# Evacuations split over two engines, squares of two frames on VectorE, no state products in block 0, idle matmuls at the start, a new order

## The chip, the cores and the metric

The kernel runs on one core of one Trainium2 chip. A core has TensorE (PE in the rows, its weight loads PEld), VectorE (DVE), ScalarE (ACT), GpSimd (POOL) and a queue engine (SP) that issues DMAs. The metric is the time of one execution on the device in microseconds (us); the median over executions counts.

## The reference: what is computed

Three stages in a row, all in fp32. First a gated linear attention over B=2, H=8, S=768, D=48, with a complex decay per position:

```python
mag = sqrt(a_re**2 + a_im**2); scale = minimum(mag, 0.999) / (mag + 1e-6)
for t in range(S):                       # state S_re, S_im: [B, H, D, D]
    S_re, S_im = ar*S_re - ai*S_im + k[t] v[t]^T, ar*S_im + ai*S_re
    y[t] = q[t] @ S_re
```

Then a mixture of experts over the 1536 tokens (y as rows of 384): a gate picks one of 8 experts, each relu(x w1) w2 with width 1024, up to a capacity. Last a network x w_in (2048 wide), a leaky relu with a slope per column, and w_out.

## The kernel before

**Attention as blocks.** The 768 positions are 6 blocks of 128, in 3 frames f of two blocks j. All logarithms and angles of the decay are summed over the positions of a frame by matmuls with triangular matrices: L_sums(f, j) and Th_sums(f, j) on TensorE, each two products of 384 columns. exps(f, j) turns the sums of logarithms into factors (ScalarE), scale(f, j) multiplies q and k with them (VectorE), phase(f, j) takes the angle to a fraction of a turn (VectorE), sin_cos(f, j) makes sine and cosine (ScalarE). Before that, the magnitude needs squares, logs, inverses, correction (ScalarE), tangent, clip_log, correct_log (VectorE) and angle (ScalarE), in four parts n: parts 0 and 1 are the two blocks of frame 0 (768 columns each), parts 2 and 3 are frames 1 and 2 (1536 columns each).

**Groups.** A block has 4 groups of four heads of one batch, so a frame has 8, numbered g. For a group: rotate(f, g) multiplies q and k with cosine and sine (VectorE, two instructions); transpose_group transposes both (TensorE, into banks TRQ and TRK); q_evacuate and k_evacuate copy these to SBUF; score_group multiplies them; mask_scores keeps the lower triangle (VectorE); apply_group multiplies the scores with v and adds q times the state from earlier blocks (the L1096 and L1099 products, 16 instructions each); add_group makes k^T v of the group for the state; state(f, u) adds it to w0 to give w1, or to w1 to give w2 (VectorE); shift_state takes w2 to the next frame. Two groups share one y, which y_evacuate(f, u) copies back. w0 of frame 0 is zero.

**Routing.** When a block's y is there, x_transpose(t), xT_evacuate(t) and tile_logits(t) make the gate's logits of 128 tokens, 12 in all, spread between the groups of frame 2. Then VectorE and TensorE route the tokens, GpSimd scatters the rows, and the experts and the network follow, bounded by TensorE. That part isn't touched.

**Order.** Each engine has its instructions in one list, written out by hand in the lines of calls: L496 to L590 for ScalarE, L778 to L885 for VectorE, L1136 to L1263 for TensorE. Engines wait for each other by counting semaphores; a wait holds everything behind it on that engine. ScalarE loads a table of functions when the kind changes (L422). ScalarE evacuates all but k of frame 0 and q of the first two groups, and squares both parts of frames 1 and 2 itself (L432, L433). One matmul call in fp32 is two instructions in the rows; a transpose is one. TensorE waits for the constants of GpSimd (`consts`) ahead of all. From frame 0 to frame 1 the last row of angles is carried: SP copies it by DMA after phase (carry_row), and carry_angle adds it on VectorE.

## Time and profile before

| | us |
|---|---|
| median of 3 runs (lowest, highest) | 519.65 (518.85, 520.82) |
| the profiled execution, its own time | 518.74 |
| its span in the profile | 516.7 |
| TensorE / VectorE / ScalarE busy over the span | 453.3 / 347.3 / 269.9 |
| attention and logits, to the first routing instruction | 146.1 |

The profile is of one execution. A view is one way of asking the trace: the table of stages gives busy time of each engine in stretches, the timeline gives instructions in order of time (start in us, duration in us, engine, line, output<-inputs, shapes, count, and in brackets how long the engine had been idle and what ended it), the groups give mean durations of equal instructions, and the chain goes back from the last instruction through what released each. A busy TensorE is pipelined: the pitch from start to start says more than the duration.

### The profile page before, as it was taken

Reading aid. Unit: us, or ns where it says so; the run is one execution under the profiler, and the core shown is the slowest. Engines: PE = TensorE matmul, PEld = TensorE weight load, DVE = VectorE, ACT = ScalarE, POOL = GpSimd, SP = SyncE. Lnnn points to the kernel's source line nnn. Section 1 sums busy time; section 2 is a strip of 40 time slices with the busy share of each in tenths; the row PEclk is TensorE's granted clock in tenths of the full one; section 3 lists DMA queues with packets and bytes.
Section 4 is the critical chain, followed back from the end, with each engine's and each line's share of the span. In section 5 each row is a group of like instructions: output and inputs, shape, how many; then the busy total and the mean of one; then the engine's idle time right before and its main releaser. Section 6 shows DMA issues by size and latency. Waiting matters only on the chain.

```text
span 516.7 us, 9892 instructions
## 1 busy us (share of the span) xinstructions
PE 453.3 (88%) x3712; PEld 409.2 (79%) x3712; DVE 347.3 (67%) x551; ACT 269.9 (52%) x425; POOL 40.1 (8%) x50
## 2 busy tenths in 40 slices
PE   0439989999940699999999989999999999999995
PEld 0227878899830499999999988999989999899985
DVE  2589898863350477777777767787747887478751
ACT  5999998564450466666666653333333333343312
POOL 3000000000037700000000000000030000200002
PEclk9969999999965699999999999999999999999999
DMA  8990000100015886667666672332333333210001
GB/s 310 421 369 2 4 3 3 3 3 3 3 31 200 277 266 196 178 204 217 204 198 198 182 225 67 110 105 91 93 122 115 99 99 108 94 68 1 0 1 63
DMA packets 27149, 63.75 MB, mean 123 GB/s; under 512 B 7894, under 2 KB 9430, under 8 KB 27100
## 3 DMA queue, kind: packets, MB, share of 16 engines
q1 hardware_dynamic: 25564, 58.34, 35.4%
q0 software_dynamic: 1536, 4.74, 2.4%
q8 instruction: 32, 0.52, 0.4%
q14 instruction: 17, 0.14, 0.1%
HBM read 58.28 MB, written 4.76 MB: 122 GB/s over the span
## 4 chain that ended last, share of the span: by engine, by line
PE 82%; DVE 5%; issue 4%; DMA 3%; POOL 3%; ACT 2%; SPq 0%; POOLq 0%; DVEq 0%; ACTq 0%
PE banks L1291 17%; PE banks L1289 17%; PE banks L1290 17%; PE banks L1299 8%; PE banks L1073 4%; PE banks L1300 4%; PE banks L1028 3%; PE banks L1096 2%; PE banks L1059 2%; POOL rows_by_slot L390 2%; PE banks L1099 2%; PE banks L1062 2%; DMA th<-a_im_rows 1%; PE banks L1109 1%; PE banks L1122 1%
## 5 line engine op out<-in xcount | busy, mean ns | idle before, releaser
L944 DVE TENSOR_TENSOR w_lo<-raw_early,w_hi 128x768 fp32r<-128x768 f32 x84 | 80.1, 957 | 30.0 <-ACT w_hi L599 29.0
L644 ACT ACTIVATE g_hi<-g_all 128x512 fp32r<-128x512 f32 x48 | 30.3, 632 | 119.0 <-DVE g_all L1001 119.0
L599 ACT ACTIVATE w_hi<-raw_early 128x768 fp32r<-128x768 f32 x84 | 70.3, 843 | 32.1 <-PE banks L1300 31.9
L1289 PE MATMUL banks<-w_hi,g_hi 128*128 128x384 f32 x192 | 65.1, 339 | 0.5 <-DVE g_lo L1003 0.5
L1291 PE MATMUL banks<-w_hi,g_lo 128*128 128x384 f32 x192 | 65.0, 339 | 0.0
L1290 PE MATMUL banks<-w_lo,g_hi 128*128 128x384 f32 x192 | 64.9, 338 | 0.0
L1299 PE MATMUL banks<-h_hi_lo,w_hi 128*128 128x448 f32 x192 | 64.0, 378 | 0.4 <-DVE h_hi_lo L964 0.4
L1003 DVE TENSOR_TENSOR g_lo<-g_all,g_hi 128x512 fp32r<-128x512 f32 x48 | 33.2, 693 | 44.2 <-ACT g_hi L644 44.2
L1289 PE MATMUL banks<-ys_hi,w_hi 128*128 128x512 f32 x144 | 56.1, 390 | 1.5 <-DVE ys_lo L978 1.5
L1291 PE MATMUL banks<-ys_hi,w_lo 128*128 128x512 f32 x144 | 57.1, 397 | 0.0
L1290 PE MATMUL banks<-ys_lo,w_hi 128*128 128x512 f32 x144 | 56.8, 394 | 0.0
L1289 PE MATMUL banks<-xs_hi,w_hi 128*128 x192 | 52.7, 275 | 0.1
L1290 PE MATMUL banks<-xs_lo,w_hi 128*128 x192 | 52.6, 274 | 0.0
L1291 PE MATMUL banks<-xs_hi,w_lo 128*128 x192 | 52.6, 274 | 0.0
L1300 PE MATMUL banks<-h_hi_lo,w_lo 128*128 128x224 f32 x192 | 50.8, 265 | 0.0
L999 DVE TENSOR_SCALAR g_neg<-banks,alpha 128x512 f32<-128x512 f32 x48 | 35.8, 747 | 7.7 <-PE banks L1291 7.6
L1299 PEld LDWEIGHTS banks<-h_hi_lo,w_hi 128*128 128x128 f32 x192 | 36.2, 189 | 3.9 <-DVE h_hi_lo L964 1.6
L1289 PEld LDWEIGHTS banks<-w_hi,g_hi 128*128 128x128 f32 x192 | 36.1, 188 | 3.4 <-DVE g_lo L1003 1.5
L1290 PEld LDWEIGHTS banks<-w_lo,g_hi 128*128 128x128 f32 x192 | 36.1, 188 | 2.0
L1289 PEld LDWEIGHTS banks<-xs_hi,w_hi 128*128 128x128 f32 x192 | 36.6, 191 | 1.0 <-issue 0.3
L399 POOL DMA_INDIRECT out_rows<-xq,tok_slot x12 | 11.8, 987 | 324.0 <-ACT xq L653 322.1
L1291 PEld LDWEIGHTS banks<-xs_hi,w_lo 128*128 128x128 f32 x192 | 36.9, 192 | 0.0
(146 smaller groups left out, 930.4 us busy)
## 6 DMA issues: line engine op xcount, KB each, us to landing
raw_early<-weights SPq DMA_DIRECT2D x84, 384.0 KB, 3.5
...
```

What stands on the lines that cost most here:

```text
L599: A(wh[:, slot, :], raw[slot], ACT.Copy).then_inc(w_hi, 1)
L644: A(gh[:, c % GBUF, :], gg[:, c % GBUF, :], ACT.Copy).then_inc(g_hi, 1)
L944: TT(wl[:, slot, :], raw[slot], wh[:, slot, :].bitcast(F32), ALU.subtract).then_inc(w_lo, 1)
L999: TS(gn[:, :], HM[c % HBUF][:, :], 0.0, alpha[:, i:i + 1], ALU.min, ALU.mult).then_inc(g_neg, 1)
L1003: TT(gl[:, c % GBUF, :], gg[:, c % GBUF, :], gh[:, c % GBUF, :].bitcast(F32), ALU.subtract).then_inc(g_lo, 1)
L1028: x = MM(to[:, b, :], lhsT=(through if j else beyond)[:, :], rhs=half(t, f, j, b), start=True, stop=True)
L1073: x = MM(SC[g % 2][:, c], lhsT=kT[:, g % 2, c], rhs=qT[:, g % 4, c], start=True, stop=True)
L1289: MM(o, lhsT=whi, rhs=mhi, start=first, stop=False)
L1290: MM(o, lhsT=whi, rhs=mlo, start=False, stop=False)
L1291: return MM(o, lhsT=wlo, rhs=mhi, start=False, stop=last)
L1299: MM(both, lhsT=whi, rhs=hs[:, slot, :, 0:n], start=first, stop=False)
L1300: return MM(o[:, 0:n], lhsT=wlo, rhs=hh[:, slot, 0:n], start=False, stop=last)
```

## The change

- Squares of parts 2 and 3 move from ScalarE to VectorE (re_im_squares). Those of parts 0 and 1 stay as they are.
- Evacuations: of 24 q, 24 k, 12 y and 12 xT, VectorE makes 8, 9, 8 and 4 (before 2, 8, 0, 0) and ScalarE the rest.
- apply_group of the first block (f = 0, j = 0, four groups) leaves out the products with the state, which is zero.
- 23 calls of idle_matmuls on TensorE: 16 ahead of all sums, one after Th_sums(0, 0), six after L_sums(0, 0). Each is four products of the identity with itself into a bank that is overwritten later. Th_sums(0, 0) now comes before L_sums(0, 0), and L_sums(0, 1) after the first transposes.
- ScalarE does part 0 to the end before part 1, with one table load more in all.
- Waits are added in rotate, shift_state, state and add_group.
- The order of all three lists is new, mainly in frames 0 and 1; add_group comes earlier in TensorE's list. The diff shows the lists up to frame 1; in the rest, too, single calls change places.

```diff
--- before.py
+++ after.py
@@ -426,12 +426,6 @@
                 act.wait_ge(a_dma[n], 32)
                 A(part(lr, n), part(th, n), ACT.Square).then_inc(im_squared, 1)
 
-            def squares(n):
-
-                act.wait_ge(a_dma[n], 32)
-                A(part(lr, n), part(th, n), ACT.Square)
-                A(part(t1, n), part(aa, n), ACT.Square).then_inc(squared_later, 1)
-
             def logs(n):
                 table(LOGS)
                 act.wait_ge(u_ready, n + 1)
@@ -495,96 +489,75 @@
 
             table(LOGS)
             square(0)
+            logs(0)
+            inverses(0)
             square(1)
-            logs(0)
+            correction(0)
+            angle(0)
             logs(1)
-            inverses(0)
             inverses(1)
-            correction(0)
+            exps(0, 0)
             correction(1)
-            angle(0)
             angle(1)
-            squares(2)
-            exps(0, 0)
+            sin_cos(0, 0)
+            logs(2)
+            q_evacuate(0, 0)
             exps(0, 1)
-            sin_cos(0, 0)
+            inverses(2)
+            k_evacuate(0, 2)
+            correction(2)
             sin_cos(0, 1)
-            logs(2)
-            inverses(2)
-            q_evacuate(0, 2)
-            correction(2)
-            squares(3)
-            q_evacuate(0, 3)
             angle(2)
+            k_evacuate(0, 3)
+            exps(1, 0)
+            k_evacuate(0, 4)
+            y_evacuate(0, 0)
             q_evacuate(0, 4)
-            exps(1, 0)
-            q_evacuate(0, 5)
-            y_evacuate(0, 0)
             exps(1, 1)
             logs(3)
             q_evacuate(0, 6)
             sin_cos(1, 0)
             q_evacuate(0, 7)
-            y_evacuate(0, 1)
             inverses(3)
             k_evacuate(1, 0)
-            q_evacuate(1, 0)
             correction(3)
-            y_evacuate(0, 2)
+            k_evacuate(1, 1)
             q_evacuate(1, 1)
-            k_evacuate(1, 1)
+            y_evacuate(0, 3)
             sin_cos(1, 1)
             k_evacuate(1, 2)
-            y_evacuate(0, 3)
             q_evacuate(1, 2)
             angle(3)
...
@@ -677,9 +650,14 @@
                 dve.wait_ge(re_squared, n + 1)
                 TT(part(t1, n), part(t1, n), part(lr, n), ALU.add).then_inc(u_ready, 1)
 
+            def re_im_squares(n):
+                dve.wait_ge(a_dma[n], 32)
+                TT(part(lr, n), part(th, n), part(th, n), ALU.mult)
+                TT(part(t1, n), part(aa, n), part(aa, n), ALU.mult).then_inc(squared_by_dve, 1)
+
             def squared_sum(n):
 
-                dve.wait_ge(squared_later, n - 1)
+                dve.wait_ge(squared_by_dve, n - 1)
                 TT(part(t1, n), part(t1, n), part(lr, n), ALU.add).then_inc(u_ready, 1)
 
             def scale(f, j):
@@ -735,6 +713,8 @@
                     dve.wait_ge(trig_ready, 2 * f + (j + 1))
                     dve.wait_ge(scaled, 2 * f + (j + 1))
                 dve.wait_ge(added, ROT_FREE + 8 * f + (g + 1 - 4))
+                if 8 * f + g >= 4:
+                    dve.wait_ge(transposed, 8 * f + (g + 1 - 4))
                 at = j * BW + b * UW + h * D
                 trig = cs[:, :, at:at + G4 * D].rearrange("p c (h d) -> p c h d", d=D)
                 for dst, src in ((qt, rows(f, j, b)), (kt, half(kk, f, j, b))):
...
@@ -742,16 +722,25 @@
                            heads(src)[:, None, h:h + G4, :].to_broadcast([P, 2, G4, D]), trig, ALU.mult)
                 x.then_inc(rot_ready, 1)
 
+            def q_evacuate(f, g):
+                dve.wait_ge(transposed, 8 * f + (g + 1))
+                if 8 * f + g >= 4:
+                    dve.wait_ge(applied, QT_FREE + 8 * f + (g + 1 - 4))
+                dve.tensor_copy(qT[:, g % 4, :], TRQ[0:DP, :]).then_inc(q_out, 1)
+
             def k_evacuate(f, g):
-                if f >= 1:
-                    return
                 dve.wait_ge(transposed, 8 * f + (g + 1))
                 dve.wait_ge(scored, KT_FREE + 8 * f + (g + 1 - 2))
                 dve.tensor_copy(kT[:, g % 2, :], TRK[0:DP, :]).then_inc(k_out, 1)
 
-            def first_q_evacuate(g):
-                dve.wait_ge(transposed, g + 1)
-                dve.tensor_copy(qT[:, g, :], TRQ[0:DP, :]).then_inc(q_out, 1)
+            def y_evacuate(f, u):
+                dve.wait_ge(applied, QT_FREE + 8 * f + (2 * u + 2))
+                dve.tensor_copy(rows(f, u // 2, u % 2), YB[:, 0:UW]).then_inc(y_out, 1)
+
+            def xT_evacuate(t):
+                dve.wait_ge(xT_made, t + 1)
+                dve.wait_ge(logits_made, XT_FREE + t + 1 - 2)
+                dve.tensor_copy(xT[:, t % 2, :], XB[:, 0:DM]).then_inc(xT_out, 1)
 
             def mask_scores(f, g):
                 dve.wait_ge(scored, KT_FREE + 8 * f + (g + 1))
@@ -764,6 +753,8 @@
                 c = slice((u % 2) * UW, (u % 2 + 1) * UW)
                 src, dst = (w0, w1) if u < 2 else (w1, w2)
                 dve.wait_ge(added, ROT_FREE + 8 * f + (2 * u + 2))
+                if f >= 1 and u < 2:
+                    dve.wait_ge(applied, QT_FREE + 8 * (f - 1) + (2 * u + 6))
                 TT(dst[:, c], UB[0:DP, 0:UW], src[:, c], ALU.add).then_inc(state_out, 1)
 
             def shift_state(f, b):
@@ -772,116 +763,138 @@
                 if b == 0:
                     dve.wait_ge(hop_ready, f + 1)
                 dve.wait_ge(state_out, U_FREE + 6 * f + (5 if b else 3))
+                dve.wait_ge(applied, QT_FREE + 8 * f + (2 * b + 2))
                 TT(heads(w0[:, c]), heads(w2[:, c]), hop[:, 1, h][:, :, None].to_broadcast([DP, H, D]),
                    ALU.mult).then_inc(state_out, 1)
 
             re_square(0)
             abs_square(0)
             re_square(1)
+            tangent(0)
+            clip_log(0)
             abs_square(1)
-            tangent(0)
+            correct_log(0)
+            re_im_squares(2)
+            phase(0, 0)
+            squared_sum(2)
             tangent(1)
-            clip_log(0)
             clip_log(1)
-            correct_log(0)
+            scale(0, 0)
+            re_im_squares(3)
+            rotate(0, 0)
+            phase(0, 1)
             correct_log(1)
-            squared_sum(2)
-            phase(0, 0)
-            scale(0, 0)
-            phase(0, 1)
-            scale(0, 1)
-            rotate(0, 0)
             rotate(0, 1)
             k_evacuate(0, 0)
-            first_q_evacuate(0)
             rotate(0, 2)
+            state(0, 0)
+            rotate(0, 3)
             k_evacuate(0, 1)
-            first_q_evacuate(1)
+            q_evacuate(0, 1)
+            scale(0, 1)
             mask_scores(0, 0)
-            k_evacuate(0, 2)
-            rotate(0, 3)
+            clip_log(2)
             mask_scores(0, 1)
+            q_evacuate(0, 2)
             tangent(2)
+            correct_log(2)
+            state(0, 1)
+            q_evacuate(0, 3)
             rotate(0, 4)
-            clip_log(2)
-            k_evacuate(0, 3)
-            correct_log(2)
-            state(0, 0)
-            mask_scores(0, 2)
-            k_evacuate(0, 4)
             rotate(0, 5)
             rotate(0, 6)
+            mask_scores(0, 2)
+            rotate(0, 7)
+            carry_angle(1, 0)
             squared_sum(3)
-            state(0, 1)
             mask_scores(0, 3)
-            carry_angle(1, 0)
+            q_evacuate(0, 5)
+            scale(1, 0)
             k_evacuate(0, 5)
-            scale(1, 0)
+            state(0, 2)
             phase(1, 0)
-            rotate(0, 7)
             k_evacuate(0, 6)
-            carry_angle(1, 1)
+            y_evacuate(0, 1)
             mask_scores(0, 4)
             mask_scores(0, 5)
-            state(0, 2)
+            k_evacuate(0, 7)
+            carry_angle(1, 1)
             rotate(1, 0)
             rotate(1, 1)
-            k_evacuate(0, 7)
-            phase(1, 1)
+            mask_scores(0, 6)
+            mask_scores(0, 7)
+            y_evacuate(0, 2)
+            q_evacuate(1, 0)
             hop_factors(1)
             rotate(1, 2)
             shift_state(0, 0)
-            mask_scores(0, 6)
...
@@ -1031,6 +1044,11 @@
             def first_frame(f):
                 return isinstance(f, int) and f == 0
 
+            def idle_matmuls():
+
+                for _ in range(4):
+                    MM(YB[:, 0:P], lhsT=ident[:, :], rhs=ident[:, :], start=True, stop=True)
+
             def L_sums(f, j):
                 pe.wait_ge(lnr_ready, parts(f, j))
                 if not first_frame(f):
@@ -1090,18 +1108,20 @@
                     pe.wait_ge(y_out, Y_FREE + 4 * f + g // 2)
                     pe.wait_ge(state_out, U_FREE + 6 * f + (b + 1 if j else -2 * (1 - b)))
                 w = w1 if j else w0
+                first = f == 0 and j == 0
                 for i in range(G4):
                     h = g % 2 * G4 + i
                     for r in ROW_HALVES:
-                        MM(YB[r, h * D:(h + 1) * D], lhsT=sc[:, g % 2, i * P + r.start:i * P + r.stop],
-                           rhs=values(f, g, i), start=True, stop=False)
-                    for r in ROW_HALVES:
+                        x = MM(YB[r, h * D:(h + 1) * D], lhsT=sc[:, g % 2, i * P + r.start:i * P + r.stop],
+                               rhs=values(f, g, i), start=True, stop=first)
+                    for r in ROW_HALVES if not first else ():
                         x = MM(YB[r, h * D:(h + 1) * D], lhsT=qT[:, g % 4, i * P + r.start:i * P + r.stop],
                                rhs=w[:, b * UW + h * D:b * UW + (h + 1) * D], start=False, stop=True)
                 x.then_inc(applied, 1)
 
             def add_group(f, g):
                 values_here(f, g)
+                pe.wait_ge(rot_ready, 8 * f + (g + 1))
                 if g % 2 == 0:
                     pe.wait_ge(state_out, U_FREE + 6 * f + (-1, 1, 2, 3)[g // 2])
                 for i in range(G4):
@@ -1133,62 +1153,85 @@
                                start=(k == 0), stop=(k == KB - 1))
                 x.then_inc(logits_made, 1)
 
+            idle_matmuls()
+            idle_matmuls()
+            idle_matmuls()
+            idle_matmuls()
+            idle_matmuls()
+            idle_matmuls()
+            idle_matmuls()
+            idle_matmuls()
+            idle_matmuls()
+            idle_matmuls()
+            idle_matmuls()
+            idle_matmuls()
+            idle_matmuls()
+            idle_matmuls()
+            idle_matmuls()
+            idle_matmuls()
+            Th_sums(0, 0)
+            idle_matmuls()
             L_sums(0, 0)
-            L_sums(0, 1)
-            Th_sums(0, 0)
+            idle_matmuls()
+            idle_matmuls()
+            idle_matmuls()
+            idle_matmuls()
+            idle_matmuls()
+            idle_matmuls()
             Th_sums(0, 1)
             transpose_group(0, 0)
+            add_group(0, 0)
+            L_sums(0, 1)
+            add_group(0, 1)
             transpose_group(0, 1)
+            add_group(0, 2)
             score_group(0, 0)
             transpose_group(0, 2)
             score_group(0, 1)
+            add_group(0, 3)
             apply_group(0, 0)
-            add_group(0, 0)
+            apply_group(0, 1)
+            score_group(0, 2)
             transpose_group(0, 3)
-            score_group(0, 2)
-            add_group(0, 1)
-            apply_group(0, 1)
+            L_sums(1, 0)
+            add_group(0, 4)
             transpose_group(0, 4)
-            L_sums(1, 0)
-            add_group(0, 2)
-            add_group(0, 3)
             score_group(0, 3)
-            transpose_group(0, 5)
+            add_group(0, 5)
             L_sums(1, 1)
             apply_group(0, 2)
+            transpose_group(0, 5)
             score_group(0, 4)
+            apply_group(0, 3)
             Th_sums(1, 0)
             transpose_group(0, 6)
-            add_group(0, 4)
-            add_group(0, 5)
-            apply_group(0, 3)
+            add_group(0, 6)
             score_group(0, 5)
+            add_group(0, 7)
             transpose_group(0, 7)
+            apply_group(0, 4)
+            apply_group(0, 5)
             score_group(0, 6)
+            score_group(0, 7)
+            transpose_group(1, 0)
             Th_sums(1, 1)
-            add_group(0, 6)
-            apply_group(0, 4)
-            transpose_group(1, 0)
-            apply_group(0, 5)
-            score_group(0, 7)
-            add_group(0, 7)
+            apply_group(0, 6)
             transpose_group(1, 1)
+            apply_group(0, 7)
             score_group(1, 0)
-            apply_group(0, 6)
+            add_group(1, 0)
             transpose_group(1, 2)
-            add_group(1, 0)
-            apply_group(0, 7)
+            add_group(1, 1)
             score_group(1, 1)
             L_sums(2, 0)
-            add_group(1, 1)
             apply_group(1, 0)
+            score_group(1, 2)
             apply_group(1, 1)
+            add_group(1, 2)
+            add_group(1, 3)
             transpose_group(1, 3)
-            add_group(1, 2)
-            score_group(1, 2)
-            add_group(1, 3)
+            apply_group(1, 2)
             L_sums(2, 1)
...
```

## Rows read from the trace of the kernel before

**Rows 1.** Table of stages: PE, PEld, DVE, ACT, POOL busy us, PEclk, DMA, GB/s.

```profile
70.00:80.00 10.00, 10.00 (x175) 9.20 (x176) 9.93 (x16) 9.16 (x13) 0.00 (x0) 1.00 0.02 4
...
130.00:140.00 10.00, 10.00 (x175) 9.03 (x176) 3.03 (x6) 4.22 (x9) 0.00 (x0) 1.00 0.01 2
```

**Rows 2.** Timeline of VectorE at the end of the logits.

```profile
146.11 0.26 DVE L896 COPY logit<-banks 128x96 f32<-128x96 f32 x1 [4.49 <-PE banks L1132]
```

**Rows 3.** Timeline at 65 to 67 us, VectorE and TensorE.

```profile
65.20 1.27 DVE L759 TENSOR_TENSOR scores<-banks,upto 128x512 f32<-128x512 f32 x2
...
66.02 1.13 PE L1073 MATMUL banks<-qT,kT 112*128 112x128 f32 x8 [1.61 <-DVE scores L759]
```

**Rows 4.** Timeline of TensorE, 92 to 98 us.

```profile
92.44 1.56 PE L1028 MATMUL banks<-th,upto_per_turn 128*128 128x384 f32 x4
...
94.80 0.32 PE L1096 MATMUL banks<-vv,scores 128*64 128x48 f32 x4
...
95.77 0.22 PE L1109 MATMUL banks<-vv,k_rot 128*64 128x48 f32 x1
...
96.33 2.05 PE L1073 MATMUL banks<-qT,kT 112*128 112x128 f32 x16
98.31 0.26 PE L1109 MATMUL banks<-vv,k_rot 128*64 128x48 f32 x1
```

**Rows 5.** Timeline of TensorE's weight loads, 19 to 42 us.

```profile
19.42 0.50 PEld L1028 LDWEIGHTS banks<-lr,after 128*128 128x128 f32 x2 [19.42 <-issue]
...
22.79 0.33 PEld L1028 LDWEIGHTS banks<-lr,upto 128*128 128x128 f32 x1 [0.31 <-issue]
23.43 0.33 PEld L1028 LDWEIGHTS banks<-lr,upto 128*128 128x128 f32 x1 [0.31 <-issue]
23.89 1.16 PEld L1028 LDWEIGHTS banks<-th,after_per_turn 128*128 128x128 f32 x4
25.18 1.16 PEld L1028 LDWEIGHTS banks<-th,upto_per_turn 128*128 128x128 f32 x4
33.97 0.69 PEld L1059 LDWEIGHTS banks<-ident,q_rot 128*112 128x112 f32 x4 [7.63 <-DVE k_rot L741]
...
38.90 1.83 PEld L1073 LDWEIGHTS banks<-qT,kT 112*128 112x128 f32 x8
40.77 0.41 PEld L1059 LDWEIGHTS banks<-ident,q_rot 128*112 128x112 f32 x4
```

**Rows 6.** Timeline of ScalarE at its start.

```profile
4.30 1.28 ACT L422 ACT_TABLE_LOAD   x1 [4.30 <-POOL prior L376]
```

**Rows 7.** Timeline of VectorE, 25 to 28 us.

```profile
25.70 0.96 DVE L711 TENSOR_SCALAR cos_sin<-banks 128x768 f32<-128x768 f32 x1 [0.30 <-PE banks L1028]
...
27.57 0.95 DVE L689 TENSOR_TENSOR xq<-xq,aa 128x768 f32<-128x768 f32 x1
```

**Rows 8.** Groups, 0 to 150 us: busy us, mean ns, idle before.

```profile
L741 DVE TENSOR_TENSOR k_rot<-kk,cos_sin 128x384 f32<-128x384 f32 x24 | 13.2, 550 | 0.0
...
L750 DVE COPY kT<-banks 112x512 f32<-112x512 f32 x8 | 5.5, 683 | 2.5 <-PE banks L1062 2.5
...
L695 DVE TENSOR_TENSOR th<-th,aa 128x1536 f32<-128x1536 f32 x2 | 3.5, 1749 | 0.0
...
L700 DVE TENSOR_SCALAR lr<-lr 128x1536 f32<-128x1536 f32 x2 | 1.9, 950 | 0.0
...
L479 ACT ACTIVATE qT<-banks 112x512 f32<-112x512 f32 x22 | 13.0, 589 | 6.9 <-PE banks L1062 6.8
```

**Rows 9.** Chain of waits: start us, us, what.

```profile
14.31 0.73 ACT aa L445
...
61.66 2.57 DMA xT<-th
```

**Rows 10.** Timeline of VectorE, 84 to 100 us, two rows with idle.

```profile
86.84 0.69 DVE L759 TENSOR_TENSOR scores<-banks,upto 128x512 f32<-128x512 f32 x1 [2.27 <-PE banks L1073]
...
94.11 0.96 DVE L711 TENSOR_SCALAR cos_sin<-banks 128x768 f32<-128x768 f32 x1 [1.05 <-PE banks L1028]
```

155 lines of the change are left out of this document (77 added, 78 removed).

## Prediction

> **What bounds the kernel now.** I read the table of stages first, since busy shares are means over stages. From 70 to 140 us TensorE is busy all the time; VectorE and ScalarE are nearly full beside it at 70 to 80 and down to a third or so at 130 to 140 [rows 1]. So the attention stage has two halves. The second is bounded by TensorE: the last logits land at 146.11 and nothing else is due before them [rows 2]. The seam is at 66.02: the timeline has TensorE idle for 1.61 us until VectorE's masked scores, and I found no idle of it after that up to the logits [rows 3]. Before the seam it is VectorE's order that sets the pace.
>
> From this follows the way to count: the end of the stage is the moment at which TensorE stops waiting, plus the work that is then left on it. What follows the logits (routing, experts, network) isn't touched, so a shift of that end is the shift of the kernel.
>
> TensorE's own prices at full clock, from start to start in the timeline [rows 4]: a running sum of four instructions and a transposed group 2.36 us together (92.44 to 94.80), an applied group of 32 instructions 0.97 (94.80 to 95.77), an added group 0.56 (95.77 to 96.33), and two score groups 1.98 (96.33 to 98.31), so 0.99 for one, which is four matmuls in eight instructions.
>
> **The idle matmuls: their price.** A call of idle_matmuls is four 128x128 products in fp32, the same shape and count as a score group but for 128 rows instead of 112. So it costs 0.99 us at full clock [rows 4] and 1.87 us at half clock (38.90 to 40.77) [rows 5]. They can start when the constants are there, at 4.30 [rows 6]. The weight loads of the first sums start 0.64 us apart (22.79 to 23.43) and after 23.89 four of them take 1.29 (to 25.18), 0.32 each: the engine ran at 1.2 GHz from its first work at 19.42 to about 23.8, and at 2.4 GHz thereafter [rows 5]. That is 4.4 us. The sixteen calls in front therefore take 4.4 us for the first 2.35 and 13.65 x 0.99 = 13.5 us for the rest, and end at 22.2. This is late: the angles that Th_sums(0, 0) needs are ready at about 15.6, by ScalarE's new order (square and logs to 9.1, table 10.4, inverses 11.9, square 12.7, correction 13.4, table 14.7, arctangent 15.6; a table load 1.28 [rows 6], 768 columns 0.74 behind one another and 0.83 behind a wait, as the chain shows them [rows 9]). TensorE takes its instructions in order, so Th_sums(0, 0) runs from 22.2 to 23.6. Bounds: if the clock is full from the start, 16 x 0.99 ends at 20.1, 2.1 earlier; if it takes as long to rise as in the second cold stretch, whose half-speed work begins at 33.97 and ends at 40.77 (6.8 us) [rows 5], it ends at 23.3, 1.1 later. I take 22.2, since that stretch has gaps and the first one has none.
> The page "TensorE: Matmul & The Clock Gate" of the Trainium skill (section "What's actually happening") says that the throttled state is the default and activity releases it. By that rule the idle calls pay: the sums, two transposed groups and a score group that ran at half speed in this trace would run at full speed, some 5 us of TensorE's time. The sum here gives them nothing, since VectorE is last in that stretch.
>
> **VectorE from there on.** One of its instructions costs its duration less about 0.08, because the next starts before it ends: two masks of 0.69 take 1.27 [rows 3]. A phase takes 1.87 (25.70 to 27.57), a scale two pieces of 0.95, so 1.73 [rows 7]; a rotation 2 x 0.47 = 0.93; an evacuation 0.61 for 512 columns, and 0.47 for 384, as a state; 1536 columns 1.67, 768 columns 0.87; a clip of 1536 columns 0.87, of 768 half of it [rows 7, 8].
> From 23.6: phase(0, 0) 1.9, squared_sum(2) 1.7, tangent(1) 0.9, clip_log(1) 0.5, scale(0, 0) 1.7, re_im_squares(3) 2 x 1.67 = 3.35. Sum 10.1: rotate(0, 0) starts at 33.7, beside 32.9 before. The two squares of frame 1, re_im_squares(2), lie at 15.3 to 18.7 while VectorE would wait for the angles anyway: nothing, as long as the idle run lasts that long.
> From 33.7 to the end of mask_scores(0, 4): 8 rotations 7.4, phases (0, 1) and (1, 0) 3.8, scales (0, 1) and (1, 0) 3.5, eight evacuations of 512 columns 4.9, three states 1.4, one y 0.5, five masks 3.0, tangent(2), correct_log(2) and squared_sum(3) 5.0, clip_log(2) and correct_log(1) 1.7, carry_angle(1, 0) 0.9. Sum 32.1: it ends at 65.8, and the trace of before has the same mask end at 65.8, too (65.20 and 0.60) [rows 3]. What is taken off VectorE there (three k evacuations) comes back as q and y evacuations and as squares.
> Does ScalarE keep up? With an added table load of 1.28 [rows 6] and without the squares the cosines of (0, 0) come at 32.8 (needed 33.7), the exponentials of (0, 1) at 40.7 (42.5), the cosines of (0, 1) at 49.5 (51.5). Slack 1 to 2 us: none is last. The carried row takes 2.57 us from phase(1, 0) [rows 9]; that ends at 64.2, so it lands at 66.8, and carry_angle(1, 1) is due at 67.0. Covered, by little.
>
> **TensorE from there on.** At 66.0 it starts apply_group(0, 4). At 66.0 in the kernel before it starts score_group(0, 6). What is then left differs by two added groups: before, add_group(0, 6) and (0, 7) are still to come, after they are done. That is 2 x 0.56 to 0.6 = 1.2 us less. I walked the rest of the order with the prices above, and TensorE has no wait: its inputs are there 0.6 to 1.5 us ahead (least at L_sums(2, 0) and Th_sums(2, 1), 0.6 us). After about 105 VectorE has time to spare again.
> **State products of block 0.** 4 groups x 16 instructions, half of 0.97 each: 1.9 us less on TensorE. All four lie before 66 us, where it waits for VectorE: nothing.
> **Evacuations moved.** 6 q, 1 k, 8 y and 4 xT go to VectorE (7 x 0.61 + 12 x 0.47 = 9.9 us), the squares add 4 x 1.67 = 6.7; ScalarE is relieved by about as much. An evacuation of 112x512 takes 683 ns on VectorE and 589 on ScalarE [rows 8]. Beyond frame 0 they lie in VectorE's gaps, which are two of 2.27 and 1.05 us between 84 and 94 [rows 10] and large ones after 105.
> The Trainium skill speaks against that part: "ScalarE is closer to PSUM, VectorE is closer to SBUF" (page "ScalarE: Activation LUTs", section "Step-by-step: what each stage is for"). The trace agrees, by 0.09 us for one evacuation. By the rule the nineteen moved copies are a loss of 1.8 us, where the sum has none because TensorE covers them.
> **New waits.** rotate waits for the transposes of four groups before, shift_state and state for applied groups, add_group for its own rotation. Each is met 1 us or more earlier by the orders above: nothing.
>
> **Sum.** 0 for VectorE's chain, -1.2 for the two groups already done. The profiled execution took 518.74 us (span 516.7), so 517.5; the median of the runs shown is 0.9 higher, 519.65, so 518.4.
>
> **Rivals.**
> *The idle run ends sooner.* If the clock is full from the start, everything from Th_sums(0, 0) on is 2.1 us earlier, because VectorE's order carries it one to one: -3.3, 516.4. For it: no row shows the pace before 19.42. Against: the first work there is ran at half pace [rows 5]. If an idle product were one instruction, like a transpose, the run would end before 15.6 and ScalarE's inverses would be last: rotate(0, 0) at 28.9, 4.8 earlier, -6.0 in all, 513.7. Against: every fp32 product written with matmul stands as two in the counts.
> *VectorE is late in frame 1 (slower than before).* From 66 to 98 its order has no gap left, where before it idled 3.3 us at two waits for TensorE [rows 10]. Now five evacuations there (y and q) each wait for a product that has just ended. If the old waits stay (3.3) and the five add 0.4 each (2.0), 5.3 us less the slack of 0.6 reach TensorE: 4.7 later, 523.1. It decides from 1.8 us of VectorE waits on, where the gain is gone.
> *The clock falls again* between 34 and 50, where TensorE has work for about three quarters of the time. L_sums(0, 1) and the groups before it then take 3.1 us more, ScalarE's slack takes 2: with what follows +1.5, 519.9.
> *It doesn't do what it says:* the state products and the clock give nothing because they aren't on the path. That is the forecast itself.
>
> **How the numbers follow.** Forecast 0.50, idle run at full clock 0.20, the one-instruction case 0.05, VectorE late 0.15, clock falls 0.10. Within 0.5% (2.6 us, about what a measurement of this kernel can tell from no change) lie the forecast but for its lower edge, the fallen clock and a mild form of the late VectorE: 0.58. Faster by more: the two cases of the shorter run and that edge, 0.28. Slower by more: 0.14. The range goes from 515.0 (the full clock, and 1.4 us that I overcharged VectorE's 42 us) to 522.0 (the long rise of the clock, +1.1, and half of the late VectorE, +2.4).
>
> **What would show it.** The start of Th_sums(0, 0) at 22.2: much earlier means the price or the clock of the idle calls was wrong. rotate(0, 0) at 33.7 without idle before it on VectorE from 23.6. The mask of (0, 4) ending at 65.8. TensorE's timeline without idle from 66 on: idle before a score or transposed group of frame 1, released by VectorE, is the slower rival. Half clock between 34 and 50 is the third. If the logits land later than 146.1 with all of these right, the pitches of TensorE have changed.

## The result and the profile after

The kernel after takes 516.34 us in the median of 8 runs (515.51 to 517.72), against 519.64 (518.21 to 520.82) of 8 runs of the kernel before. The ratio is 0.9938 with an interval of [0.9923, 0.9953]: 3.3 us, or 0.6%, faster. The prediction was 518.4 with a range of 515.0 to 522.0: the time lies in the range, but the gain of 3.3 us is over two and a half times the 1.2 forecast.

The profiled execution took 516.6 us, its span is 514.6, so 2.1 less than before. The page gives busy time of each engine over the span:

```profile
span 514.6 us, 10165 instructions
PE 471.6 (92%) x3832; PEld 428.6 (83%) x3832; DVE 363.7 (71%) x574; ACT 257.8 (50%) x403; POOL 40.2 (8%) x50
```

The table of stages (busy us of PE, PEld, DVE, ACT, POOL with the number of instructions, granted clock, DMA share, GB/s):

```profile
34.00:38.00 4.00, 3.00 (x24) 1.92 (x23) 3.97 (x8) 3.38 (x4) 0.00 (x0) 0.77 0.89 343
38.00:42.00 4.00, 4.00 (x47) 2.77 (x46) 2.58 (x7) 2.89 (x6) 0.00 (x0) 0.80 0.03 9
...
70.00:80.00 10.00, 10.00 (x142) 8.37 (x141) 9.93 (x16) 9.45 (x13) 0.00 (x0) 1.00 0.01 2
130.00:140.00 10.00, 10.00 (x194) 9.23 (x193) 5.21 (x9) 1.69 (x3) 0.00 (x0) 1.00 0.01 3
```

TensorE is full in both late stretches, as before [rows 1]; at 130 to 140 work has gone from ScalarE to VectorE (5.21 and 1.69, before 3.03 and 4.22). The first pair shows the granted clock between 34 and 42 us. It is below full there, though higher than in the kernel before:

```profile
34.00:38.00 4.00, 2.53 (x11) 2.14 (x12) 2.89 (x6) 3.97 (x4) 0.00 (x0) 0.50 0.93 360
38.00:42.00 4.00, 4.00 (x26) 3.97 (x25) 2.27 (x5) 3.97 (x4) 0.00 (x0) 0.65 0.01 3
```

Timeline of VectorE and TensorE (start us, us, engine, line, what, idle before and what ended it) at the seam and at the last logits:

```profile
65.15 1.28 DVE L748 TENSOR_TENSOR scores<-banks,upto 128x512 f32<-128x512 f32 x2
65.89 0.32 PE L1115 MATMUL banks<-vv,scores 128*64 128x48 f32 x4
...
143.76 0.26 DVE L909 COPY logit<-banks 128x96 f32<-128x96 f32 x1 [4.52 <-PE banks L1152]
```

The seam is where it was (65.15, before 65.20 [rows 3]), and TensorE has no idle before its row at 65.89. The logits come at 143.76, before at 146.11 [rows 2]: 2.35 us earlier. Nearly all of it was gained behind the seam, where 77.87 us are left (65.89 to 143.76), before 80.09 (66.02 to 146.11).

One thing is different at the seam itself. Before, TensorE stood idle there for 1.61 us. Now the last wait that its timeline shows ahead of the seam is this one:

```profile
52.43 0.26 PE L1129 MATMUL banks<-vv,k_rot 128*64 128x48 f32 x1 [0.44 <-DVE k_rot L721]
```

From 52.4 us on TensorE is full, and VectorE is full beside it. I keep the word seam for the mask at 65.15, so that kernels can be compared, but TensorE bounds the stage from somewhat earlier on (e3_state_back below shows it).

**The beginning.** TensorE's timeline:

```profile
4.34 16.71 PE L1050 MATMUL banks<-ident 128*128 128x128 f32 x128 [4.34 <-POOL prior L376]
20.89 1.46 PE L1041 MATMUL banks<-th,after_per_turn 128*128 128x384 f32 x4
22.18 1.05 PE L1050 MATMUL banks<-ident 128*128 128x128 f32 x8
23.07 1.46 PE L1041 MATMUL banks<-lr,after 128*128 128x384 f32 x4
...
33.40 0.65 PE L1077 MATMUL banks<-ident,q_rot 128*112 128x128 f32 x4 [2.22 <-DVE k_rot L721]
...
36.12 2.89 PE L1041 MATMUL banks<-lr,upto 128*128 128x384 f32 x4 [0.18 <-DVE lr L683]
```

A call of idle_matmuls is 0.89 us where it stands alone (22.18 to 23.07), not 0.99, so the angle sums run from 20.9 and not from 22.2. Then TensorE idles, the mean granted clock from 34 to 38 us is 0.77 (table above), and L_sums(0, 1) at 36.12 takes 2.89 us, where four instructions of the same shape took 1.46 at 20.89.

VectorE's timeline, with the two ends of that:

```profile
22.38 0.96 DVE L689 TENSOR_SCALAR cos_sin<-banks 128x768 f32<-128x768 f32 x1 [3.91 <-PE banks L1041]
...
32.33 0.55 DVE L721 TENSOR_TENSOR q_rot<-xq,cos_sin 128x384 f32<-128x384 f32 x1
...
39.96 0.56 DVE L758 TENSOR_TENSOR w<-banks,w 112x384 f32<-112x384 f32 x1 [1.42 <-PE banks L1131]
```

rotate(0, 0) starts at 32.33 (forecast 33.7). state(0, 0) at 39.96 has waited 1.42 us for add_group(0, 1), which stands behind L_sums(0, 1) on TensorE. So 1.3 us gained are 1.4 lost, and the seam doesn't move.

**Behind the seam.** The chain of waits, before (L1073 score groups, L1028 sums) and after (L1091, L1041), in pieces of start us, us, what:

```profile
72.05 1.09 PE banks L1073 x8
74.75 0.89 PE banks L1073 x8
80.35 1.29 PE banks L1028 x4
87.40 1.49 PE banks L1028 x4
```

```profile
75.26 1.09 PE banks L1091 x8
79.64 1.29 PE banks L1041 x4
87.17 1.49 PE banks L1041 x4
88.66 0.89 PE banks L1091 x8
```

A score group has two prices in both kernels. It is 0.89 behind products whose weights fill 112 or 128 columns (scores, transposes, sums) and 1.09 behind those whose weights are 64 or 48 columns (apply, add, logits: "128*64" in the timeline); a sum is 1.29 or 1.49. A change back from narrow to full weights costs 0.20 us. By the lists of calls TensorE makes 32 such changes behind the seam before and 28 after.

### The profile page after: what moved, and what is told of

Same layout as the page of the kernel before. It is cut to its first block, busy times and chain, and to the rows that moved or that the text cites. A ratio compares the mean times of both kernels' runs of the same rounds, so it can differ in the third digit from the quotient of the medians.

```text
span 514.6 us, 10165 instructions
## 1 busy us (share of the span) xinstructions
PE 471.6 (92%) x3832; PEld 428.6 (83%) x3832; DVE 363.7 (71%) x574; ACT 257.8 (50%) x403; POOL 40.2 (8%) x50
## 4 chain that ended last, share of the span: by engine, by line
PE 79%; DVE 5%; issue 3%; POOL 3%; DMA 1%; ACT 1%; DVEq 0%; POOLq 0%; SPq 0%; ACTq 0%
PE banks L1332 16%; PE banks L1334 16%; PE banks L1333 16%; PE banks L1342 8%; PE banks L1091 4%; PE banks L1343 4%; PE banks L1041 2%; PE banks L1115 2%; POOL rows_by_slot L390 2%; PE banks L1077 2%; PE banks L1118 2%; PE banks L1080 2%; PE banks L1129 1%; PE banks L1326 1%; PE banks L1142 1%
```

## The experiments

Each kernel was timed in three rounds beside the kernel before. Three moments of its profile are in this table: rotate(0, 0), the mask that is the seam, and the last logits. The last columns are the median and the ratio to the kernel before as it was timed beside each.

| kernel | rotate(0, 0) | seam | logits | seam to logits | us | ratio |
|---|---|---|---|---|---|---|
| before | 32.90 | 65.20 | 146.11 | 80.91 | 519.64 | |
| after | 32.33 | 65.15 | 143.76 | 78.61 | 516.34 | 0.9938 [0.9923, 0.9953] |
| e1_no_idle | 31.48 | 63.42 | 142.02 | 78.60 | 515.20 | 0.9914 [0.9887, 0.9942] |
| e2_ten_ahead | 32.23 | 63.85 | 142.46 | 78.61 | 515.65 | 0.9928 [0.9904, 0.9953] |
| e4_keep_clock | 32.52 | 63.84 | 142.45 | 78.61 | 515.57 | 0.9912 [0.9884, 0.9940] |
| e5_ten_and_clock | 32.19 | 65.98 | 145.22 | 79.24 | 516.88 | 0.9931 [0.9909, 0.9954] |
| e3_state_back | 32.88 | 65.92 | 144.85 | 78.93 | 516.35 | 0.9946 [0.9929, 0.9962] |
| e8_fewer_switches | 32.31 | 64.95 | 141.69 | 76.74 | 513.63 | 0.9895 [0.9878, 0.9911] |
| e9_evac_back | 32.28 | 64.95 | 143.71 | 78.76 | 517.03 | 0.9958 [0.9943, 0.9972] |
| e11_sp_first | 28.31 | 59.63 | 138.24 | 78.61 | 510.83 | 0.9844 [0.9828, 0.9861] |
| e6_before_adds | 33.01 | 65.79 | 145.50 | 79.71 | 518.13 | 0.9982 [0.9966, 0.9999] |
| e7_before_idle | 32.84 | 64.15 | 145.06 | 80.91 | 518.92 | 0.9993 [0.9977, 1.0010] |
| e10_squares_act | 31.89 | 63.22 | 141.83 | 78.61 | 514.84 | 0.9926 [0.9900, 0.9953] |
| e12_all | 28.31 | 59.64 | 136.38 | 76.74 | 509.74 | 0.9827 [0.9798, 0.9856] |

Read the column from seam to logits first. It is 78.61 within 0.01 us in six kernels whose seams lie between 59.6 and 65.2 us. So the way to count of the prediction holds: the time is where TensorE stops waiting, plus the work left on it. Three kernels with the same order of TensorE behind the seam stand a little off: e9_evac_back (78.76), e3_state_back (78.93) and e5_ten_and_clock (79.24), where VectorE waits 0.90 us for the carried row at 98.64.

The moments are sharper than the medians. Behind the seam they repeat to 0.01 us in those six; ahead of it they don't: four kernels with the same order up to rotate(0, 0) have it between 32.28 and 32.52, and a fifth (e3_state_back) at 32.88. Of the kernels made from the kernel after, only e8_fewer_switches, e11_sp_first and e12_all have ratios whose intervals lie apart from its own. For the others a difference to it rests on the moments of one profile each. The rest of the span, from the logits on, which no kernel changes, varied from 369.8 to 371.6 us over these fourteen profiles, and one profile's time can't be told from another's within that.

**Without the idle matmuls.** All 23 calls are taken out.

```diff
-            idle_matmuls()      (23 times)
```

> The changed kernel without any of the 23 calls of idle_matmuls. In the trace of the changed kernel the 16 calls in front end at 20.89 us, while the angles that Th_sums(0, 0) needs are ready at about 15.6, and VectorE works without a gap from phase(0, 0) at 22.38 to 38.5. Theory 1 (the idle run delays the start of VectorE's chain, and the clock is worth little in that stretch): Th_sums(0, 0) starts at 15.6 at half clock, rotate(0, 0) at about 28.5 instead of 32.3, 3.8 us earlier; the transposes and sums of block 0 at half clock take about 1.5 us of it back; 2.3 us faster than the changed kernel, 514.0 us. Rival (the idle calls pay, because they keep the clock at 2.4 GHz until the real work comes): without them sums, transposes and scores of block 0 run at half clock and VectorE waits for them; slower than the changed kernel by 1 to 5 us, 517.5 to 521.

Measured: 515.20 us, and the logits at 142.02, 1.7 earlier than with the calls. TensorE and VectorE:

```profile
15.69 2.90 PE L1041 MATMUL banks<-th,after_per_turn 128*128 128x384 f32 x4 [15.69 <-ACT th L449]
...
26.40 0.96 DVE L667 TENSOR_TENSOR xq<-xq,aa 128x768 f32<-128x768 f32 x1 [2.81 <-SPq L299]
```

The angles are there at 15.69, as the prediction had it (15.6). At half clock the sums take twice as long, and yet they come earlier: the calls in front had held them for 5.2 us (15.69 to 20.89). Little of that arrives. The second row is a surprise: scale(0, 0) waits 2.81 us for SP, so rotate(0, 0) is only 0.85 us earlier than in the kernel after, and not 3.8. The other 0.9 comes from the wait at state(0, 0), which is 0.52 us instead of 1.42, because L_sums(0, 1) takes 2.11 us instead of 2.89. The measured time lies between the theory (514.0) and the rival (517.5 or more). By the medians the calls cost 1.1 us, but the two intervals overlap; by the logits it is 1.7.

**Ten calls in front instead of sixteen.**

```diff
-            idle_matmuls()      (6 of the 16 ahead of Th_sums(0, 0))
```

> The changed kernel with 10 calls of idle_matmuls ahead of the sums instead of 16. In the changed kernel 20 instructions run at half clock to 8.6 us and the rest 0.113 us apart, so 10 calls should end at about 15.6, just when the angles are ready. Theory 1: Th_sums(0, 0) at 15.7 instead of 20.9; VectorE's phase(0, 0) at 18.4 (behind its squares of part 2) instead of 22.4; rotate(0, 0) at about 28.5 instead of 32.3; the logits end 3.6 us earlier; 512.7 us. Rival: ScalarE becomes last (its inverses end at 21.35 in any case, and its exponentials, angle and cosines follow from there) and holds the rest of the chain: 1 us or less faster than the changed kernel, 515.5.

Measured: 515.65, and rotate(0, 0) at 32.23, not at 28.5. The sums did start early (15.78) and at full clock (1.46 us). VectorE then stops:

```profile
27.14 0.96 DVE L667 TENSOR_TENSOR xq<-xq,aa 128x768 f32<-128x768 f32 x1 [3.82 <-SPq L299]
```

What SP does meanwhile, in its timeline of the kernel after:

```profile
17.90 9.18 SPq L295 DMA_DIRECT2D raw_early<-weights  x6
```

SP announces that q, k and v of frame 0 have landed (`qkv_here`, L299), and only after it has issued six loads of expert weights, which hold it until 27.1. In the kernel after scale(0, 0) starts at 27.25, right behind, so this bound stood exactly where VectorE's own order came to it and was visible in no idle time. Neither theory had it; the rival's 515.5 is met for another reason than its own.

The logits are 1.3 us earlier all the same. With rotate(0, 0) where it was, this comes from the clock: TensorE's transposes ran at half clock (granted 0.50 from 30 to 34 us), but the clock was up again during L_sums(0, 1), and from 38 to 42 us it was 1.00 (0.80 in the kernel after).

```profile
36.21 1.80 PE L1041 MATMUL banks<-lr,upto 128*128 128x384 f32 x4
38.66 0.56 DVE L758 TENSOR_TENSOR w<-banks,w 112x384 f32<-112x384 f32 x1 [0.21 <-PE banks L1131]
```

L_sums(0, 1) took 2.89 us in the kernel after, and VectorE's wait at state(0, 0) was 1.42; here they are 1.80 and 0.21.

**The clock kept up.** Two idle calls after Th_sums(0, 1) and one after transpose_group(0, 0), into the first bank of scores.

```diff
             Th_sums(0, 1)
+            idle_in_scores()
+            idle_in_scores()
             transpose_group(0, 0)
+            idle_in_scores()
             add_group(0, 0)
```

> The changed kernel with three more calls of idle matmuls, into a scores bank that is still free: two between Th_sums(0, 1) and transpose_group(0, 0), where TensorE waits 2.2 us for the rotation, and one after transpose_group(0, 0). In the changed kernel the granted clock is 0.77 at 34 to 38 us and 0.80 at 38 to 42, L_sums(0, 1) takes 2.89 us instead of 1.46, ScalarE waits for it until 39.11 and VectorE stands idle 1.42 us before state(0, 0). Theory (the fallen clock costs these 1.4 us): with the clock kept up L_sums(0, 1) takes 1.4 us, VectorE's idle time goes, all that follows is 1.2 to 1.4 us earlier; 515.0 us. Rival (VectorE waits there for other reasons, or the time is given back later where TensorE alone is bound): no change, 516.3.

Measured: 515.57 us, logits at 142.45, 1.3 earlier than after. TensorE and its clock:

```profile
36.32 1.56 PE L1041 MATMUL banks<-lr,upto 128*128 128x384 f32 x4
```

```profile
34.00:38.00 4.00, 3.85 (x42) 2.80 (x41) 3.97 (x7) 3.60 (x5) 0.00 (x0) 1.00 0.93 353
```

The sums of logarithms take 1.56 and not 2.89, and the 1.42 us of VectorE's wait at state(0, 0) are gone. That was the fallen clock, as the theory had it. (The ratio, 0.9912 with an interval up to 0.9940, doesn't separate this kernel from the kernel after.)

**Both.**

```diff
-            idle_matmuls()      (6 of the 16)
+            idle_in_scores()    (3, as above)
```

> Both edits together: 10 idle calls in front and three more around transpose_group(0, 0). Theory: the two add up, since one moves the start of VectorE's chain and the other takes a hole out of it: 3.6 + 1.3 = 4.9 us faster than the changed kernel, 511.4 us. Rival (ScalarE is last from then on, since its slack was 1 to 2 us): no faster than the better of the two alone, 512.7.

Measured: 516.88, logits at 145.22. Both expectations missed by 4 us or more. TensorE:

```profile
33.26 1.10 PE L1082 MATMUL banks<-ident,q_rot 128*112 128x128 f32 x4 [4.07 <-DVE k_rot L721]
34.16 1.06 PE L1085 MATMUL banks<-ident,k_rot 128*112 128x128 f32 x4
35.01 1.91 PE L1055 MATMUL banks<-ident 128*128 128x128 f32 x8
37.87 2.27 PE L1041 MATMUL banks<-lr,upto 128*128 128x384 f32 x4
```

TensorE ran dry early, waited 4.07 us for VectorE, which waited for SP, and lost its clock. The idle call meant to keep it then took 1.91 us in front of the sums, and state(0, 0) waited 2.38 us. Only the three calls tell this kernel from e2_ten_ahead, whose seam lies at 63.85: they made it 2.13 us later. An idle call behind a long wait, with the clock already down, was a cost and no help. By the ratio (0.9931) the kernel is as fast as the kernel after.

**The state products of block 0 back.**

```diff
-                first = f == 0 and j == 0
+                first = False
```

> The changed kernel with the state products of block 0 back (32 matmul calls on zeros, 64 instructions). Theory, as in the prediction: they lie before 66 us, where TensorE waits for VectorE, so they cost next to nothing. Looked at closely, the groups (0, 2) and (0, 3) lie at 57 to 60.2 us, where TensorE's order is without idle up to Th_sums(1, 0); 1.0 us later there makes phase(1, 0) some 0.4 us later: 0.0 to 0.5 slower than the changed kernel, 516.3 to 516.8. Rival: all of it is on the path, half of four applied groups of 1.07, 1.9 to 2.1 us slower, 518.3.

Measured: 516.35, the ratio 0.9946 against 0.9938 for the kernel after: the same within the intervals. In its profile the logits are 1.1 later. A part of that is not the products': SP's announcement was late in that execution, and VectorE waited for it.

```profile
27.80 0.96 DVE L667 TENSOR_TENSOR xq<-xq,aa 128x768 f32<-128x768 f32 x1 [0.66 <-SPq L299]
```

TensorE's starts, here and in the kernel after, separate the two. At the first product of apply_group(0, 2) this kernel is 0.26 us late (57.28 and 57.02). Then come the products of the groups (0, 2) and (0, 3):

```profile
61.32 1.56 PE L1041 MATMUL banks<-th,upto_per_turn 128*128 128x384 f32 x4
66.98 0.32 PE L1115 MATMUL banks<-vv,scores 128*64 128x48 f32 x4
```

In the kernel after these two rows stand at 60.13 and 65.89. So it is 1.19 late behind the two groups, 1.09 late at the seam and 1.09 late at the logits: of some 0.93 us of products 0.83 came through. Those of the first two groups (45 to 47 us) did not: ahead of them and at apply_group(0, 2) the delay is the same 0.25. The rival, that the 1.9 us of products come back in full, is out. But they aren't free either: 0.8 us by the profile, more than the 0 to 0.5 expected. The ratio is too coarse to show it.

**Eighteen evacuations of frames 1 and 2 back to ScalarE.**

```diff
-            q_evacuate(1, 0)    (on VectorE; with it 3 more q, 4 k, 6 y, 4 xT)
+            q_evacuate(1, 0)    (the same 18 calls on ScalarE)
```

> The changed kernel with the eighteen evacuations of frames 1 and 2 that VectorE makes (4 q, 4 k, 6 y, 4 xT) back on ScalarE; frame 0 and TensorE's order stay. Theory: from 66 us on TensorE is never late, so who evacuates doesn't matter: 516.3, within 0.4. Rival 1 (VectorE is too full from 66 to 100 and delays TensorE by pieces that the timeline doesn't show): 1 us faster. Rival 2 (split evacuation is what keeps TensorE fed, since ScalarE alone hands q and k over later): 1 to 2 us slower, with idle of TensorE before transposed and score groups.

Measured: 517.03, and the logits at 143.71, as after (143.76). VectorE gets idle time back (1.53 us at 92, for one), and TensorE's timeline shows none. From seam to logits it is 0.15 more. The median is 0.7 us above that of the kernel after, within the intervals. So the split is worth 0.15 us by the profile, and nothing that the ratios can tell.

**Fewer changes of weight width.** Frame 2 of TensorE's list in another order, with 8 changes from narrow to full weights from x_transpose(1) on instead of 16; a few evacuations change places with it.

```diff
             tile_logits(0)
-            x_transpose(2)
             add_group(2, 1)
+            x_transpose(2)
             score_group(2, 0)
...
             apply_group(2, 2)
+            apply_group(2, 3)
+            tile_logits(7)
+            x_transpose(8)
             transpose_group(2, 6)
-            apply_group(2, 3)
-            x_transpose(8)
-            transpose_group(2, 7)
-            tile_logits(7)
             x_transpose(9)
...
```

> The changed kernel with another order of TensorE's list in frame 2 only: added groups, applied groups and logits follow one another where they can, so that there are 8 changes from products of 64 columns of weights (apply, add, logits) to full ones (scores, transposes, sums) from x_transpose(1) on, where there were 16. The y of (2, 1) and the xT of 8 are evacuated one place earlier; the work is the same. Both traces show a score group at 1.09 us behind a group of the first kind and at 0.89 behind one of the second, a sum at 1.49 and 1.29, a transposed group at 1.02 and 0.88. Theory: a change costs about 0.17 us, so this is 8 x 0.17 = 1.4 us faster than the changed kernel, 514.9; the logits at 142.4 instead of 143.8. Rival (the difference lies in how ends are modelled, or the new order makes TensorE wait for evacuations): no faster, 516.3 or more.

Measured: 513.63, ratio 0.9895. From seam to logits 76.74 us instead of 78.61: 1.87 for eight changes, 0.23 each, with the same products.

```profile
141.69 0.26 DVE L909 COPY logit<-banks 128x96 f32<-128x96 f32 x1 [3.89 <-PE banks L1152]
```

That is somewhat more than expected, and none of it lies ahead of the seam. TensorE shows no wait in that stretch in either kernel, so it is not a wait that went.

**SP announces first.** With ten calls in front and the clock kept:

```diff
+            sp.wait_ge(qkv_dma[0], 48)
+            sp.sem_inc(qkv_here, 1)
             for i in range(AHEAD):
                 sp.dma_start(raw[i], w_in[i, :, :]).then_inc(w_dma[i], 16)
...
-            for f in range(NF):
+            for f in range(1, NF):
```

> The kernel with 10 idle calls ahead and three more around transpose_group(0, 0), and with one move on SP: it waits for q, k and v of frame 0 and announces them before it issues the six loads of weights, not after. With 10 calls VectorE stood idle 3.8 us before scale(0, 0), until SP's count at 27.1, right after SP had issued the last of these loads (16.99 and 10.06 us later). Theory: the data had long landed and only SP's order held the count back; then scale(0, 0) starts at about 23.4, rotate(0, 0) at 28.5, all that follows comes 3.8 us earlier and the clock stays up through L_sums(0, 1): logits at 142.45 - 3.8 = 138.7, 511.8 us. Rival (the transfers themselves land at 26 to 27, all sixteen DMA engines being full until 37): as with the late count, 515.6 to 516.9.

Measured: 510.83, logits at 138.24 (expected 138.7). Against e5_ten_and_clock this differs by SP's order alone, and is 7.0 us earlier at the logits and 0.0087 lower in the ratio (4.5 us):

```profile
23.24 0.95 DVE L669 TENSOR_TENSOR xq<-xq,aa 128x768 f32<-128x768 f32 x1
...
28.31 0.55 DVE L723 TENSOR_TENSOR q_rot<-xq,cos_sin 128x384 f32<-128x384 f32 x1
```

```profile
29.39 0.65 PE L1084 MATMUL banks<-ident,q_rot 128*112 128x128 f32 x4 [0.19 <-DVE k_rot L723]
...
32.11 1.56 PE L1043 MATMUL banks<-lr,upto 128*128 128x384 f32 x4
```

VectorE has 0.30 us of idle time (at 78.69) from there to 87 us, TensorE waits 0.19 us where it had waited 4.07, and its clock stays.

**The added groups alone, in the kernel before.** add_group(0, 6) and (0, 7) go ahead of score_group(0, 6), with state(0, 2) earlier on VectorE so that they can.

```diff
+            state(0, 2)
             carry_angle(1, 1)
             mask_scores(0, 4)
             mask_scores(0, 5)
-            state(0, 2)
...
             transpose_group(0, 7)
+            add_group(0, 6)
+            add_group(0, 7)
             score_group(0, 6)
             Th_sums(1, 1)
-            add_group(0, 6)
...
-            add_group(0, 7)
```

> The kernel before with one step of the change alone: state(0, 2) goes ahead of carry_angle(1, 1) on VectorE, and add_group(0, 6) and (0, 7) go ahead of score_group(0, 6) on TensorE, into the 1.6 us in which it waits for the masked scores until 66.02. Theory, as in the prediction: work that is moved into that hole no longer stands behind it; 2 x 0.56 = 1.1 us faster than before. Rival (the hole is needed for the transfer of the carried row and moves with it, or VectorE's state comes later than the hole): no change.

Measured: 518.13, ratio 0.9982 [0.9966, 0.9999], 0.9 us. From seam to logits 79.71 instead of 80.91, so 1.20. The seam itself is 0.6 later. VectorE waits for the carried row as long as before (1.11 us, before 1.16); it is the row that comes later:

```profile
64.92 0.95 DVE L721 SCALAR_TENSOR_TENSOR th<-xT,th 1x768 f32<-1x768 f32 x1 [1.11 <-DMA xT<-th]
65.79 1.27 DVE L759 TENSOR_TENSOR scores<-banks,upto 128x512 f32<-128x512 f32 x2
```

phase(1, 0) starts 0.17 later than before (59.85 and 59.68), and the DMA of the row took 3.0 us from its issue to landing instead of 2.6. The edit touches neither.

**The idle matmuls alone, in the kernel before.** Fourteen calls ahead of L_sums(0, 0).

```diff
+            idle_matmuls()      (14 times)
             L_sums(0, 0)
             L_sums(0, 1)
```

> The kernel before with 14 calls of idle_matmuls ahead of L_sums(0, 0) and nothing else; they should end at about 19.0 us, just ahead of the sums at 19.45. Theory: the sums then run at full clock and end some 2 us earlier, but ScalarE comes to the exponentials only at 24.9, behind its squares and a table load, and VectorE to the phase behind squared_sum at 25.4: 0 to 0.3 us faster than before. Rival (idle matmuls pay by themselves): the 2 us of the sums go through to the end, 517.2 to 517.7.

Measured: 518.92, ratio 0.9993 [0.9977, 1.0010]. The time says nothing measurable. Its profile has the seam 1.05 earlier:

```profile
63.27 0.95 DVE L721 SCALAR_TENSOR_TENSOR th<-xT,th 1x768 f32<-1x768 f32 x1 [0.25 <-DMA xT<-th]
```

Before, the same instruction waited 1.16 us for the carried row. The first two sums took 2.90 and 2.23 us before and 1.46 and 1.45 here, but phase(1, 0) is only 0.14 us earlier (59.54 and 59.68). The rest of the 1.05 is the row's DMA, from issue to landing, before and here:

```profile
xT<-th SPq DMA_DIRECT2D x1, 3.0 KB, 2.6
xT<-th SPq DMA_DIRECT2D x1, 3.0 KB, 1.7
```

So the idle calls gave at most 0.14 us, inside the 0 to 0.3 expected, and 0.9 is the transfer of one small row, whose time differs from profile to profile.

**The squares of part 3 on ScalarE,** in the idle time it has after inverses(1).

```diff
             inverses(1)
+            squares(3)
...
-            re_im_squares(3)
```

> The changed kernel with the squares of part 3 (frame 2) on ScalarE, in its idle time of 3.3 us before the exponentials of (0, 0); VectorE makes those of part 2 only. Theory: VectorE has 3.35 us less ahead of rotate(0, 0), which then waits for the cosines at 31.45 instead of standing at 32.33: 0.9 us faster, 515.4, logits at 142.9. Rival 1 (ScalarE is pushed and hands over the exponentials later): no gain. Rival 2 (VectorE's whole 3.35 us come through): 513.0.

Measured: 514.84, logits at 141.83, 1.9 earlier than after. VectorE and ScalarE:

```profile
31.89 0.56 DVE L728 TENSOR_TENSOR q_rot<-xq,cos_sin 128x384 f32<-128x384 f32 x1 [2.78 <-ACT cos_sin L474]
```

```profile
22.30 1.48 ACT L432 ACTIVATE lr<-th 128x1536 f32<-128x1536 f32 x1 [0.98 <-DMA th<-a_im_rows]
```

VectorE sheds 3.35 us of squares and gets 0.44 of it: ScalarE's squares begin at 22.30, when the rows of a have landed, and with their 2.9 us ahead of them the cosines become last. The other 1.4 come from TensorE: it waited 1.73 us instead of 2.22 before the first transposes, kept the clock (1.00 from 34 to 38), and state(0, 0) didn't wait.

**All of it:** e11_sp_first with the order of e8_fewer_switches.

> The kernel with SP's announcement first, 10 idle calls ahead and the clock kept, and the order of frame 2 with fewer changes between kinds of products. Theory: the two gains lie in different stretches (before 60 us and after 100 us) and add up: logits at 138.2 - 2.0 = 136.2, 508.8 us. Rival (with TensorE 4 us earlier, VectorE and ScalarE are late in frame 2 for the tighter order): 509.5 to 510.8, with idle of TensorE after 100 us.

Measured: 509.74, ratio 0.9827 [0.9798, 0.9856], the fastest of all.

```profile
136.38 0.26 DVE L911 COPY logit<-banks 128x96 f32<-128x96 f32 x1 [3.89 <-PE banks L1159]
```

Its seam is that of e11_sp_first, its work behind it that of e8_fewer_switches (76.74): in the moments the two gains add up. The median lies 0.9 above the 508.8 expected, in the rival's range, but TensorE shows none of the rival's idle time after 100 us. The interval overlaps that of e11_sp_first.

## Why the prediction was right and wrong

**Right: the bound and the way to count.** The stage ends when TensorE stops waiting plus what is left. The column from seam to logits shows it. The moment itself moved, though: in the new order TensorE's last wait is at 52.4, not at 66. TensorE had no wait for VectorE in frame 1: the slower rival was wrong. The 1.8 us of waits from which it decides never came: VectorE's one wait of over 0.3 us between 66 and 98 is 0.58.

**Right: VectorE's chain.** 32.1 us were forecast from rotate(0, 0) to the end of mask_scores(0, 4). The trace has 32.33 to 65.75, so 33.4, of which 1.42 is the wait at state(0, 0): 32.0. The 10.1 us ahead of it were 9.95 (22.38 to 32.33).

**Right in the main: the added groups.** Forecast 1.2, and 1.20 in e6_before_adds between seam and logits. It has one change of width fewer as well, 31 for 32, so the groups alone are 1.0.

**Right: the evacuations, priced at nothing.** e9_evac_back has the logits 0.05 us apart. The Trainium skill says (page "ScalarE: Activation LUTs", section "Step-by-step: what each stage is for") that ScalarE is closer to PSUM. The copies here agree (512 columns took 589 ns on ScalarE and 683 on VectorE), but it decided nothing here, because TensorE covers them. The prediction's 1.8 us of loss by that rule was also too high: it took the difference of a 512-column copy for all nineteen, and twelve have 384 columns, where it is 0.07 us (551 ns on VectorE in the kernel after, 485 on ScalarE in the kernel before). That gives 1.5.

**Wrong: state products "before 66 us, where it waits for VectorE: nothing".** That held for two of the four groups. The other two lie at 57 to 60 us, where TensorE no longer waits, and e3_state_back shows 0.8 us for them. The forecast of the seam didn't suffer, since VectorE's own chain ended at the same moment.

**Wrong: the idle call at 0.99.** It was taken from two score groups behind an apply or add group, 1.98 for both [rows 4], which contained one change of width (1.09 + 0.89). Idle calls follow full weights and take 0.89. Over the 13.65 calls at full clock that is 1.4 us; Th_sums(0, 0) was 1.3 early. The term for the rising clock was right: the first 20 instructions, at half speed, took from 4.34 to about 8.8, the 4.4 us that were forecast.

**Wrong: "clock falls again" was a rival with 0.10.** It came true at 34 to 42 us, and was priced about right (1.5). e4_keep_clock shows what it cost: 1.3. This cancelled the error before, so the forecast of the seam (65.8) was right by two errors of opposite sign.

**Wrong: one price for each kind of product.** This is the step by which the forecast gain was too small. The sum has -1.2 for the two added groups and, by one price for each kind of product, nothing else behind the seam; the term for the order was missing. That a price depends on what stands ahead was in the trace, and I hadn't looked for it. The kernel after has four changes fewer behind the seam. Of the 2.30 us less between seam and logits 1.0 are the two added groups and 0.8 to 0.9 are four changes at 0.20 to 0.23; 0.4 to 0.5 stay open. e8_fewer_switches, which alters little else, shows that such changes are paid for on the path. No run separates the width of the weights from the halves of the array into which the narrow products write (ROW_HALVES); the two change together in every group here.

The page "TensorEngine Tiling (Array Packing)" of the Trainium skill (section "Tiling Modes", "Key Properties") says that changing the tiling mode drains TensorE; it gives no figure. The runs are in line with it and put 0.20 to 0.23 us on a change here; that a drain is the reason no trace shows.

**Not foreseen: SP.** It didn't enter the forecast's time, since in the kernel after VectorE came to scale(0, 0) at 27.25, when SP had just announced its inputs at 27.1. (SP's loads took 8.7 to 10.1 us from profile to profile, so where it is last, scale(0, 0) starts anywhere from 26.40 to 27.80.) But it is why fewer idle matmuls brought so little, and why the rival of 513.7 couldn't have come true as I worked it out: rotate(0, 0) at 28.9 would have needed scale(0, 0) at 23.8, 3.3 us before the announcement. That the measured median meets the 516.4 of the other rival is chance: the clock was not full from the start.

**The idle matmuls.** The prediction gave them nothing and no loss. By the moments they are a small loss in this order, of 1.3 us for six of them and 1.7 for all. They do hold sums whose inputs are there at 15.7 until 20.9, but SP's announcement hides most of that: 0.1 and 0.85 us of it arrive. The rest, 1.2 and 0.9 us, is the clock. With the calls it is full at 33 us, has fallen when L_sums(0, 1) comes (2.89 us), and is up again only behind it; without them it is down at 33 and up again during these sums (1.80 and 2.11 us). That the last six calls end at 29.7, too early to carry the clock over the wait, is why. The Trainium skill says (page "TensorE: Matmul & The Clock Gate", section "What's actually happening") that activity releases the clock. The runs agree (the same sums 1.46 against 2.90 us). Worth something was what lay on the path: three calls around the first transposes, 1.3 us.

**What is left.** The logits came 2.35 earlier and the span was 2.1 shorter, but the medians differ by 3.3, with an interval of 2.4 to 4.0. The other 0.9 shows in no trace: the part behind the logits took 370.6 and 370.8 us in the two profiles. It lies within that part's scatter from execution to execution and stays open. The 2.35 us themselves carry a chance, too: before, the seam hangs on the DMA of the carried row, which took 2.6 us in that profile, 1.7 in e7_before_idle and 3.0 in e6_before_adds. After, VectorE doesn't wait for it there.
